# Folded weight product in quarters over all attention steps, four load buffers, and an earlier last-stage load

## The chip, the cores and the metric

The kernel runs on one core of a Trainium2 chip. The metric is the device time of one execution in microseconds (us), here the median of three runs. Engines are named as the profile names them: PE (matrix products), DVE and ACT (element-wise work), POOL (GpSimd), SP (the queue that issues the DMAs).

## The reference

A decaying causal attention over 8 batches of 8 heads, 576 positions and head size 64, then two three-layer networks on the 4608 resulting tokens:

```
scores = scale * q @ k.T
ret    = scores * Dmat            # Dmat = gamma_head ** (i - j) for i >= j, else 0
x      = (ret @ v), heads side by side            # 4608 x 512
h      = max(max(x @ w1, x @ w2), x @ w3)         # 512 -> 768
x2     = h @ w_out                                # 768 -> 512
a, b   = x2 @ u1, x2 @ u2                         # 512 -> 1024
out    = ((a * b) @ u3) @ uo                      # 1024 -> 1024 -> 512
```

All inputs and outputs are 32-bit floats.

## The kernel before, in words

**Numbers.** Each large product is made from operands split into a high part (a cast, on ACT: `chi`, `whi`, `u3hi`, `uohi`) and a low part (the rest, on DVE: `clo`, `wlo`, `u3lo`, `uolo`). Three matmuls hi*hi, hi*lo and lo*hi go into one sum. The two layers after the product a*b are one: the kernel multiplies u3 by uo itself while attention runs (the folded weight product, `wcst` and `wcd`), and the last stage uses the result.

**Attention** takes 32 steps, each for one batch and two heads. A step n has `scores(n)` (16 + 4 small matmuls), `sum_state(n)`, and for step n-1 `query_state` and `values`. DVE weighs the scores (`probs`, L709 and L713) and makes the running state (L725, L728). POOL scales values and queries (`vdec`, `qdec`, L499). ACT copies the result out (`xst`, L582), and SP stores it to `xd`. The inputs of a step come in two loads of 576 KB, `qks` (two buffers) and `vks` (three). The folded product is eight blocks of 24 matmuls (L912 to L914), one in every second step from step 3 to step 17, between `scores` and `query_state`. Beside that, weights 0 to 4 of the first network stage are loaded, summed (POOL) and split within attention, and so are all seven blocks of the first token tile.

**The network stages** B, C, I, O (512 to 768, 768 to 512, 512 to 1024, 1024 to 512) take six token tiles each. A tile is cut into 2x2 blocks and multiplied by seven products P1 to P7 in place of eight; for it POOL makes four sums of token blocks (`raw`) and four of weight blocks (`wraw`). The loop variable `it` counts units, that is one weight for one tile: B has 54 (it 0 to 53), C 12, I 48 (it 66 to 113), O 12 (it 114 to 125). In iteration `it` PE runs in this order: P1(it), P5(it-1), P4(it-1), P6(it), P3(it-1), P2(it), P7(it). Every product first waits for what its operands need: the low part of its token block (`c_lo`) in the first unit of a tile, the low parts of its weight (`w_lo`) in the first tile of a stage. ACT copies P1's bank (`s`), P6's (`u`) and P7's (`w`) out of the accumulator; DVE adds P2, P3 and P5 to them.

**Order.** All engines run fixed lists. The tables HI_STD, HI_CI, HI_IO (ACT) and LO_STD, LO_CI, LO_IO (DVE) say after which point of an iteration each of a tile's seven blocks is split, around the end of one tile ("end") and the first unit of the next ("next"). W_LOAD_AT, W_SUM_AT, W_SPLIT_AT, RAW_AT and T_AT give the iteration at which SP, POOL and the splitters take up a weight or a tile. W_FREE and SLOT_FREE say which product must be done before a memory range is used again. The weights of stage O are numbers 19 and 20 (units it 114 and 115 for the first tile), its first tile is number 18; those of stage B are 0 to 8.

## Time and profile before

| | before |
|---|---|
| median of three runs | 1333.28 us (1332.85 to 1336.16) |
| profiled execution, its own time | 1333.16 us |
| its span | 1331.4 us |
| PE busy | 1259.7 us (95%) |
| DVE, ACT, POOL busy | 803.4, 459.7, 452.3 us |
| granted PE clock, mean | 0.982 |
| attention, to PE's first product of stage B | 235.5 us |

PE is busy nearly all the time, so the time can only fall where PE waits or where its clock is lowered. A row of the timeline has a start, a duration, the engine, the line, the operation, written tile and read tiles, and in brackets how long the engine had been idle before and what ended that.

### The profile page before, as it was taken

To read this page: it belongs to the slowest core of one execution; us is meant where nothing else is said; L and a number is where in the kernel's file an instruction comes from. 1 tells how busy PE (TensorE), PEld (TensorE's weight loads), DVE (VectorE), ACT (ScalarE), POOL (GpSimd) and SP (SyncE) were. 2 spreads that over 40 slices of the span, in tenths; PEclk is the share of its full clock that TensorE was granted. 3 is DMA by queue.
4 is the path that set the end of the run, shared out by engine and by line. 5 is a ranking of instruction groups with operands and counts; after the bars stand their busy time and mean duration, and the time that the engine had idled before them with its cause. 6 is when DMAs were issued, how large, how long until landed. Compare 5 with 4: busy or idle time off the path is not lost.

```text
span 1331.4 us, 20535 instructions
## 1 busy us (share of the span) xinstructions
PE 1259.7 (95%) x8032; PEld 1235.0 (93%) x8032; DVE 803.4 (60%) x1194; ACT 459.7 (35%) x707; POOL 452.3 (34%) x248
## 2 busy tenths in 40 slices
PE   6999878999999999999999999999999998499999
PEld 5888867999999999999899999999999997499999
DVE  5555668656455555548889677454535537756762
ACT  2112112433333232325455444232323323344442
POOL 2333566602020202006598562202012007635550
PEclk8999988999999999999999999999999999799999
DMA  8778786302020202031655541313313133334441
GB/s 312 235 239 288 252 286 223 133 29 95 25 95 31 89 31 90 31 137 54 224 180 176 174 157 53 109 48 101 104 58 102 52 130 120 130 137 148 155 142 66
DMA packets 82929, 174.37 MB, mean 131 GB/s; under 512 B 8976, under 2 KB 57488, under 8 KB 82832
## 3 DMA queue, kind: packets, MB, share of 16 engines
q1 hardware_dynamic: 82832, 173.05, 37.9%
q8 instruction: 64, 1.05, 0.3%
q14 instruction: 33, 0.27, 0.1%
HBM read 109.58 MB, written 63.44 MB: 130 GB/s over the span
## 4 chain that ended last, share of the span: by engine, by line
PE 74%; DMA 10%; DVE 9%; issue 4%; POOL 1%; SPq 1%; ACT 1%; DVEq 0%; POOLq 0%
PE ps L944 23%; PE ps L945 23%; PE ps L946 23%; DVE clo L699 3%; DMA vks<-vk 3%; DMA u3raw<-u3T 2%; DVE wlo L699 2%; DMA x2d<-h 2%; DMA gd<-h 1%; PE ps L890 1%; PE ps L875 1%; PE ps L900 1%; DVE state L728 1%; DVE probs L709 1%; POOL qdec L499 1%
## 5 line engine op out<-in xcount | busy, mean ns | idle before, releaser
L944 PE MATMUL ps<-chi,whi 128*128 128x384 f32 x2016 | 678.7, 337 | 32.4 <-DVE wlo L699 15.3
L945 PE MATMUL ps<-clo,whi 128*128 128x384 f32 x2016 | 676.4, 336 | 0.0
L946 PE MATMUL ps<-chi,wlo 128*128 128x384 f32 x2016 | 676.3, 335 | 0.0
L499 POOL TENSOR_TENSOR raw<-raw,raw 128x768 f32<-128x768 f32 (+2 forms) x96 | 273.3, 2866 | 536.7 <-DMA raw<-xd 222.0
L944 PEld LDWEIGHTS ps<-chi,whi 128*128 128x128 f32 x2016 | 380.7, 189 | 37.9 <-issue 18.6
L945 PEld LDWEIGHTS ps<-clo,whi 128*128 128x128 f32 x2016 | 380.9, 189 | 0.0
L946 PEld LDWEIGHTS ps<-chi,wlo 128*128 128x128 f32 x2016 | 380.7, 189 | 0.0
L699 DVE TENSOR_TENSOR clo<-raw,chi 128x768 fp32r<-128x768 f32 (+2 forms) x168 | 259.5, 1567 | 16.5 <-ACT chi L622 16.1
L622 ACT CAST chi<-raw 128x768 fp32r<-128x768 f32 (+2 forms) x168 | 180.7, 1081 | 93.8 <-PE ps L946 86.6
L689 ACT COPY w<-ps 128x384 f32<-128x384 f32 x126 | 60.8, 482 | 253.7 <-PE ps L946 252.2
L675 ACT COPY u<-ps 128x384 f32<-128x384 f32 x126 | 60.8, 482 | 168.1 <-PE ps L946 166.6
L816 DVE TENSOR_TENSOR h<-ps,u 128x384 f32<-128x384 f32 x66 | 36.7, 556 | 122.3 <-PE ps L946 122.3
L789 DVE TENSOR_TENSOR h<-ps,w 128x384 f32<-128x384 f32 x66 | 36.7, 556 | 119.9 <-PE ps L946 97.3
L656 ACT COPY s<-ps 128x384 f32<-128x384 f32 x126 | 60.7, 482 | 69.5 <-PE ps L946 69.0
L499 POOL TENSOR_TENSOR wraw<-w,wraw 128x256 f32<-128x256 f32 (+2 forms) x21 | 23.1, 1102 | 177.0 <-DMA w<-wC 80.4
L789 DVE TENSOR_TENSOR w<-ps,w 128x384 f32<-128x384 f32 x60 | 33.4, 556 | 82.4 <-PE ps L946 82.4
L699 DVE TENSOR_TENSOR wlo<-wraw,whi 128x768 fp32r<-128x768 f32 (+4 forms) x42 | 80.9, 1926 | 2.9 <-ACT whi L607 2.7
L499 POOL TENSOR_TENSOR qdec<-qks,qtab 128x512 f32<-128x512 f32 x32 | 42.0, 1314 | 77.3 <-PE ps L890 77.3
L582 ACT COPY xst<-ps 128x576 f32<-128x576 f32 x32 | 20.4, 639 | 132.0 <-PE ps L900 132.0
L816 DVE TENSOR_TENSOR u<-ps,u 128x384 f32<-128x384 f32 x60 | 33.3, 555 | 53.3 <-PE ps L946 53.3
L667 ACT COPY h<-ps 128x384 f32<-128x384 f32 x66 | 31.7, 480 | 96.3 <-PE ps L946 82.2
L499 POOL TENSOR_TENSOR vdec<-vks,vtab 128x512 f32<-128x512 f32 x32 | 42.6, 1330 | 46.0 <-DMA vks<-vk 45.2
(41 smaller groups left out, 917.1 us busy)
## 6 DMA issues: line engine op xcount, KB each, us to landing
qks<-qk SPq DMA_DIRECT2D x32, 576.0 KB, 4.4
vks<-vk SPq DMA_DIRECT2D x32, 576.0 KB, 6.0
gd<-h SPq DMA_DIRECT2D x96, 192.0 KB, 1.9
raw<-gd SPq DMA_DIRECT2D x24, 768.0 KB, 7.2
hd<-h SPq DMA_DIRECT2D x72, 192.0 KB, 1.9
raw<-hd SPq DMA_DIRECT2D x24, 576.0 KB, 5.7
raw<-xd SPq DMA_DIRECT2D x24, 384.0 KB, 5.4
x2d<-h SPq DMA_DIRECT2D x48, 192.0 KB, 2.5
```

Of the source, the lines that this page charges most:

```text
L499: return nc.gpsimd.tensor_tensor(out_, a, b, op)
L622: nc.scalar.copy(chi[st][pos][:, :, :], raw_block(tau, pos)[:, :, :]).then_inc(c_hi, 1)
L656: nc.scalar.copy(sbuf_s[it % 2][:, :], ps[:, X[it % 2], 0:N]).then_inc(s_made, 1)
L667: nc.scalar.copy(H[1][0][:, :], ps[:, X[g % 2], 0:N]).then_inc(copied21, 1)
L675: nc.scalar.copy(sbuf_u[it % 2][:, :], ps[:, X[it % 2], 0:N]).then_inc(u_made, 1)
L689: nc.scalar.copy(sbuf_w[it % 2][:, :], ps[:, X[it % 2], 0:N]).then_inc(w_made, 1)
L699: return nc.vector.tensor_tensor(out_, whole, hi.bitcast(f32), ALU.subtract)
L789: nc.vector.tensor_tensor(to[:, :], ps[:, Z[g % 2], 0:N], sbuf_w[g % 2][:, :], ALU.add).then_inc(sum22, 1)
L816: nc.vector.tensor_tensor(to[:, :], ps[:, Z[g % 2], 0:N], sbuf_u[g % 2][:, :], ALU.add).then_inc(sum12, 1)
L944: nc.tensor.matmul(to, w1, x1, start=(start and k == 0), stop=False, skip_group_check=True)
L945: nc.tensor.matmul(to, w1, x2, start=False, stop=False, skip_group_check=True)
L946: last = nc.tensor.matmul(to, w2, x1, start=False, stop=(k == KH[st] - 1), skip_group_check=True)
```

## The change

The folded product no longer comes in eight blocks but in 32 quarters of 6 matmuls: one in each step from 2 to 31, and the last two in step 32. The splits of u3 and uo and the copies out are spread to match. `qks` and `vks` get four buffers each and are loaded three steps ahead, `qdec` gets two buffers. The memory for this comes from moving things: the `vks` buffers lie where token blocks 4 to 6 of the first tile go, so these are split in iteration 0 of stage B; and only weights 0 and 1 are prepared within attention, while 2 to 8 are loaded, summed and split in iterations 0 to 6. DVE makes the state after the extra splits of a step, not before. In the last stage, tile 18 is loaded at iteration 107 in place of 110 and its first two sums stand at 109 in place of 112, weights 19 and 20 stand otherwise too, at other addresses. In stages C and O, block 6 of a tile has one buffer in place of two and is loaded last, apart from the other three, and these three are issued after two of the stores of the iteration, not before. The tables for the splits are spread by one or two points.

```
-HI_IO = {("end", "s"): [0], ("end", "u"): [1], ("end", "p2"): [2], ("next", "p5"): [3],
-         ("next", "p3"): [4, 5, 6]}
-LO_STD = {("end", "21"): [0], ("end", "11"): [1, 2], ("next", "start"): [3], ("next", "22"): [4],
-          ("next", "21"): [5], ("next", "12"): [6]}
...
-LO_IO = {("end", "21"): [0], ("end", "11"): [1, 2], ("next", "22"): [3], ("next", "12"): [4, 5],
-         ("next", "11"): [6]}
+HI_IO = {("end", "s"): [0], ("end", "u"): [1], ("end", "p3"): [2], ("end", "p2"): [3],
+         ("next", "p5"): [4], ("next", "p3"): [5, 6]}
+LO_STD = {("end", "21"): [0], ("end", "12"): [1], ("end", "11"): [2], ("next", "22"): [3],
+          ("next", "21"): [4], ("next", "12"): [5], ("next", "11"): [6]}
...
+LO_IO = {("end", "21"): [0], ("end", "12"): [1], ("end", "11"): [2, 3], ("next", "22"): [4],
+         ("next", "11"): [5, 6]}
...
-    O: [(112, P4), (112, P3), (113, P2), (113, P5), (113, P3), (113, P3), (113, P3)],
+    O: [(111, P3), (112, P3), (112, P3), (113, P2), (113, P5), (113, P3), (113, P3)],
...
-          19: ((109, P3), 18), 20: ((111, P3), 0)}
+          19: ((107, P3), 0), 20: ((110, P3), 18)}
-W_LOAD_AT = {6: 0, 7: 1, 8: 2, 9: 49, ... 18: 69, 20: 112}
-W_SUM_AT = {5: 0, 6: 1, 7: 2, 8: 3, 9: 50, ... 19: 111, 20: 113}
-W_SPLIT_AT = {wi: it + 1 for wi, it in W_SUM_AT.items()}
+W_LOAD_AT = {2: 0, 3: 0, 4: 0, 5: 1, 6: 2, 7: 3, 8: 4, 9: 49, ... 18: 69, 19: 109, 20: 112}
+W_SUM_AT = {2: 0, 3: 1, 4: 2, 5: 3, 6: 4, 7: 5, 8: 6, 9: 50, ... 19: 110, 20: 113}
+W_SPLIT_AT = {wi: it + (wi >= FIRST_W[C]) for wi, it in W_SUM_AT.items()}
...
-        _a = {C: 48, I: None, O: 110}[_st]
-        T_AT[_tau] = {C: (50, 51), I: (65, 65), O: (112, 113)}[_st]
+        _a = {C: 48, I: None, O: 107}[_st]
+        T_AT[_tau] = {C: (50, 51), I: (65, 65), O: (109, 110)}[_st]
...
-WC_AT = {3 + 2 * kb: kb for kb in range(FT2)}
+WC_FROM = 2
+def quarters(n):
+    if n == NP:
+        return range(NP - WC_FROM, QUARTERS)
+    return range(n - WC_FROM, n - WC_FROM + 1) if n >= WC_FROM else ()
+U3_LOAD = {max(4 * kb - 2, 0): kb for kb in range(1, FT2)}
+U3_HI = {max(4 * kb, 1): kb for kb in range(FT2)}
+U3_LO = {max(4 * kb + 1, 1): kb for kb in range(FT2)}
+UO_AT = {1: 0, 2: 1, 3: 2, 4: 3}
+P1_W_LOAD = {8: 0, 10: 1}
+P1_W_SUM = {10: 0, 12: 1}
+P1_RAW = 12
+P1_T = {15: 0, 16: 1, 17: 2, 18: 3}
+P1_HI = {18: 0, 19: 1, 20: 2, 22: 3}
...
             def load_qk(n):
-                if n >= 2:
-                    sp.wait_ge(scored, n - 1)
-                    sp.wait_ge(q_decayed, n - 1)
+                if n >= 4:
+                    sp.wait_ge(scored, n - 3)
+                    sp.wait_ge(q_decayed, n - 3)
             def load_vk(n):
-                if n >= 3:
-                    sp.wait_ge(valued, n - 2)
+                if n >= 4:
+                    sp.wait_ge(valued, n - 3)
...
-                if 2 <= wi <= 5:
+                if 2 <= wi <= 8:
+                    sp.wait_ge(valued, NP)
                     sp.wait_ge(wc_done, FT2)
...
+            def load_raw_rest(tau):
+                sp.wait_ge(c_lo, 7 * tau)
+                load_raw_block(tau, 6)
...
             for it in range(G + 1):
-                if it in RAW_AT:
-                    load_raw(RAW_AT[it])
+                tau = RAW_AT.get(it)
+                two_parts = tau is not None and tau // TILES in (C, O) and tau % TILES
+                if tau is not None and not two_parts:
+                    load_raw(tau)
                 g = it - 1
                 if g >= 0 and ends(g):
...
                         store(g, 1, 0)
+                        if two_parts:
+                            load_raw(tau)
                         sp.wait_ge(sum12, g + 1)
                         store(g, 0, 1)
...
+                if two_parts:
+                    load_raw_rest(tau)
...
+                    elif tau == O * TILES:
+                        pool.wait_ge(prod, DONE[(108, P3)])
...
                 if tau == 0:
-                    if pos == 6:
-                        act.wait_ge(valued, 30)
+                    if pos > 3:
+                        act.wait_ge(valued, NP)
...
+            def wc_quarter(i):
+                kb, part = divmod(i, 4)
+                if part == 0:
+                    pe.wait_ge(u3_lo, kb + 1)
+                    if kb:
+                        pe.wait_ge(wc_out, kb)
...
             for n in range(STEPS):
                 if n < NP:
                     scores(n)
-                if n in WC_AT:
-                    wc_block(WC_AT[n])
+                for i in quarters(n):
+                    wc_quarter(i)
```

**PE in attention.** First before: the end of a block (the last of its 24 matmuls), the rest of that step, and the step behind it, which has none.

```order
L914 MATMUL ps<-uohi_230,u3lo_236 128x512
L890 MATMUL ps<-qdec_249,state_250 128x128 x3
L890 MATMUL ps<-qdec_249,state_250 128x64
L875 MATMUL ps<-vdec_248,vks2_243 128x128 x4
L900 MATMUL ps<-probs_244,vks1_242 64x128 x8
L900 MATMUL ps<-probs_244,vks1_242 64x64 x2
L860 MATMUL ps<-qks_240 128x128 x8
L865 MATMUL ps<-qks_240 128x64 x2
L890 MATMUL ps<-qdec_249,state_250 128x128 x3
L890 MATMUL ps<-qdec_249,state_250 128x64
L875 MATMUL ps<-vdec_248,vks0_241 128x128 x4
```

And now: one step of the changed kernel, the first with a quarter.

```order
L875 MATMUL ps<-qks2_240 128x128 x8
L880 MATMUL ps<-qks2_240 128x64 x2
L930 MATMUL ps<-uohi_228,u3hi1_232 128x512
L932 MATMUL ps<-uolo_229,u3hi1_232 128x512
L934 MATMUL ps<-uohi_228,u3lo1_234 128x512
L930 MATMUL ps<-uohi_228,u3hi1_232 128x512
L932 MATMUL ps<-uolo_229,u3hi1_232 128x512
L934 MATMUL ps<-uohi_228,u3lo1_234 128x512
L905 MATMUL ps<-qdec1_252,state_253 128x128 x3
L905 MATMUL ps<-qdec1_252,state_253 128x64
L890 MATMUL ps<-vdec_250,vks2_244 128x128 x4
L915 MATMUL ps<-probs_246,vks1_243 64x128 x8
```

Every step from 2 on now has six matmuls of the folded product in it, where every second step had 24 or none.

**ACT where stage B begins.** Before, from the last token block of tile 0 to the end of iteration 1; `s0`, `u0`, `w0` belong to iteration 0, `s1` to iteration 1.

```order
L622 CAST chi0_6_62<-raw0_6_55 128x768
L656 COPY s0_223<-ps 128x384
L675 COPY u0_225<-ps 128x384
L689 COPY w0_227<-ps 128x384
L656 COPY s1_224<-ps 128x384
L667 COPY h10_221<-ps 128x384
L675 COPY u1_226<-ps 128x384
L607 CAST whi5_155<-wraw5_157 128x768
```

And now, from the last copy of the folded product on:

```order
L619 COPY wcst_237<-ps 128x512
L673 COPY s0_221<-ps 128x384
L642 CAST chi0_4_60<-raw0_4_53 128x768
L642 CAST chi0_5_61<-raw0_5_54 128x768
L692 COPY u0_223<-ps 128x384
L642 CAST chi0_6_62<-raw0_6_55 128x768
L627 CAST whi2_141<-wraw2_143 128x768
L706 COPY w0_225<-ps 128x384
L627 CAST whi2_141<-wraw2_143 128x1024
L673 COPY s1_222<-ps 128x384
```

Three token casts and both casts of weight 2 have come between the copies that PE waits for in iterations 0 and 1.

**POOL ahead of stage O.** The sums of weights 19 and 20 and of tile 18's token blocks, before:

```order
L499 TENSOR_TENSOR wraw19_213<-w21_19_214,wraw19_213 128x512
L499 TENSOR_TENSOR wraw19_213<-wraw19_213,w21_19_214 128x512
L499 TENSOR_TENSOR wraw19_213<-wraw19_213 128x512 x2
L499 TENSOR_TENSOR raw3_4_117<-raw3_3_116,raw3_0_113 128x1536
L499 TENSOR_TENSOR raw3_1_114<-raw3_6_119,raw3_4_117 128x1536
L499 TENSOR_TENSOR wraw20_217<-w21_20_218,wraw20_217 128x512
```

And now:

```order
L517 TENSOR_TENSOR raw3_4_116<-raw3_3_115,raw3_0_112 128x1536
L517 TENSOR_TENSOR raw3_1_113<-raw3_6_118,raw3_4_116 128x1536
L517 TENSOR_TENSOR wraw19_211<-w21_19_212,wraw19_211 128x512
L517 TENSOR_TENSOR wraw19_211<-wraw19_211,w21_19_212 128x512
L517 TENSOR_TENSOR wraw19_211<-wraw19_211 128x512 x2
L517 TENSOR_TENSOR raw3_3_115<-raw3_6_118,raw3_3_115 128x1536
L517 TENSOR_TENSOR raw3_5_117<-raw3_2_114,raw3_1_113 128x1536
L517 TENSOR_TENSOR wraw20_215<-w21_20_216,wraw20_215 128x512
```

Weight 20's sums now stand last, behind all four token sums; before, two token sums stood behind them.

## Rows read from the trace of the kernel before

**Rows 1.** What PE waited for, first 300 us (total, times, longest).
```profile
PE ps L875 <- POOL vdec L499: 14.9, 8, 5.8
```

**Rows 2.** PE timeline in attention.
```profile
15.97 1.21 PE L900 MATMUL ps<-probs,vks 128*64 128x128 f32 x20
21.27 2.08 PE L860 MATMUL ps<-qks 64*128 64x128 f32 x16 [4.09 <-DMA qks<-qk]
...
68.12 1.16 PE L860 MATMUL ps<-qks 64*128 64x128 f32 x16
72.50 1.16 PE L860 MATMUL ps<-qks 64*128 64x128 f32 x16
...
87.86 1.16 PE L860 MATMUL ps<-qks 64*128 64x128 f32 x16
94.77 1.00 PE L890 MATMUL ps<-qdec,state 128*128 128x128 f32 x8
97.78 1.16 PE L860 MATMUL ps<-qks 64*128 64x128 f32 x16
```

**Rows 3.** DMA in 0 to 240 us.
```profile
DMA packets 27518, 62.18 MB, mean 259 GB/s; under 512 B 2823, under 2 KB 15968, under 8 KB 27495
```

**Rows 4.** The page: DMA issues, size, median us from issue to landing.
```profile
vks<-vk SPq DMA_DIRECT2D x32, 576.0 KB, 6.0
raw<-gd SPq DMA_DIRECT2D x24, 768.0 KB, 7.2
```

**Rows 5.** Windows in attention; the last two numbers: DMA share, GB/s.
```profile
56.00:60.00 4.00, 3.94 (x52) 3.61 (x52) 2.35 (x10) 1.13 (x2) 2.55 (x2) 1.00 0.90 292
184.00:188.00 4.00, 1.54 (x7) 1.54 (x8) 0.00 (x0) 0.00 (x0) 2.86 (x4) 0.50 1.04 412
```

**Rows 6.** Timelines of SP, POOL, ACT at stage B's start.
```profile
237.23 0.37 SPq L384 DMA_DIRECT2D wraw<-wB  x1
...
241.37 0.74 POOL L499 TENSOR_TENSOR wraw<-w,wraw 128x256 f32<-128x256 f32 x1 [6.49 <-DMA w<-wB]
244.27 0.73 POOL L499 TENSOR_TENSOR wraw<-w,wraw 128x256 f32<-128x256 f32 x1
...
236.92 0.48 ACT L656 COPY s<-ps 128x384 f32<-128x384 f32 x1
241.93 0.48 ACT L656 COPY s<-ps 128x384 f32<-128x384 f32 x1 [0.56 <-PE ps L946]
248.54 1.05 ACT L607 CAST whi<-wraw 128x1024 fp32r<-128x1024 f32 x1
```

**Rows 7.** PE timeline in stage C, at two tile starts.
```profile
702.59 0.45 PE L944 MATMUL ps<-chi,whi 128*128 128x384 f32 x1 [1.29 <-DVE h L789]
...
726.06 0.45 PE L944 MATMUL ps<-chi,whi 128*128 128x384 f32 x1 [1.33 <-DVE h L789]
```

**Rows 8.** ACT timeline, `s` of iterations 109, 110, 116, 117 and `w` of 115.
```profile
1082.22 0.48 ACT L656 COPY s<-ps 128x384 f32<-128x384 f32 x1 [0.56 <-PE ps L946]
1089.50 0.48 ACT L656 COPY s<-ps 128x384 f32<-128x384 f32 x1 [0.56 <-PE ps L946]
...
1176.64 0.48 ACT L689 COPY w<-ps 128x384 f32<-128x384 f32 x1 [0.54 <-PE ps L946]
1178.72 0.48 ACT L656 COPY s<-ps 128x384 f32<-128x384 f32 x1 [0.22 <-PE ps L946]
...
1193.28 0.48 ACT L656 COPY s<-ps 128x384 f32<-128x384 f32 x1 [1.60 <-PE ps L946]
```

**Rows 9.** PE timeline, waits between stages I and O.
```profile
1101.90 0.59 PE L944 MATMUL ps<-chi,whi 128*128 128x384 f32 x1 [2.04 <-DVE h L789]
...
1152.12 0.66 PE L944 MATMUL ps<-chi,whi 128*128 128x384 f32 x1 [9.86 <-DVE wlo L699]
...
1166.12 0.66 PE L944 MATMUL ps<-chi,whi 128*128 128x384 f32 x1 [5.43 <-DVE wlo L699]
```

**Rows 10.** The chain of waits after the row at 1101.90 (start, us).
```profile
1105.05 0.32 PE ps L944
```

**Rows 11.** DVE and POOL timelines around stage O's start and later.
```profile
1135.06 4.56 DVE L699 TENSOR_TENSOR clo<-raw,chi 128x1536 fp32r<-128x1536 f32 x1
...
1158.64 0.56 DVE L789 TENSOR_TENSOR h<-ps,w 128x384 f32<-128x384 f32 x1 [6.67 <-PE ps L946]
1175.03 5.26 DVE L699 TENSOR_TENSOR clo<-raw,chi 128x1536 fp32r<-128x1536 f32 x3
...
1186.71 16.96 POOL L499 TENSOR_TENSOR raw<-raw,raw 128x1536 f32<-128x1536 f32 x4 [24.55 <-DMA raw<-gd]
```

240 lines of the change are left out of this document (112 added, 128 removed).

## The prediction

> **What bounds the kernel now.** I read first what PE waited for, then PE's timeline where it waited. PE is the bound: the table of times has it busy for 95% of the span, so I looked only for its gaps and its slow stretches. Three places have them: attention (to 237 us), stage C (small), and the passage from stage I to stage O. Elsewhere PE hardly pauses, and an iteration takes 1089.50 - 1082.22 = 7.28 us in stage I and 1193.28 - 1178.72 = 14.56 us in stage O [rows 8].
>
> In attention PE waited mostly for POOL's scaled values, 14.9 us [rows 1], which waited for `vks`, and once 4.09 us for `qks` [rows 2]. A step without a block takes 72.50 - 68.12 = 4.38 us. A step with one takes 97.78 - 87.86 = 9.92, so a block costs 5.54, a quarter of it 1.39 [rows 2]. If PE never waited, 32 steps and 8 blocks would take 140.2 + 44.3 = 184.5 us; they take 237.
>
> Between I and O, from the `s` copy of iteration 109 to the `w` copy of 115, 94.42 us pass [rows 8]. Undisturbed, from the two paces (a product is a seventh of an iteration, 1.04 and 2.08): four iterations of I, 29.12; six products of I and one of O, 8.32; four products of O and three of I, 11.44; six products of O, 12.48. Sum 61.36, so 33.1 us are lost. Two waits for weight 20's low parts are 15.3 of it [rows 9]. DVE is late there because its work runs slow beside POOL: a `clo` of 128x1536 took 4.56 us, while three of the same took 5.26 together (1.75 each) when POOL was idle [rows 11]. The `clo`s come ahead of the `wlo` in its list.
>
> **Attention.** Removed are the waits for loads. `vks` takes 6.0 us to land [rows 4]; it is now issued two full steps and a part ahead, over 12 us, so only bandwidth can make it late. The first steps: values(0) started at 15.97 and, with the 1.1 us that it lasts, step 2 can start at 17.1, where it waited 4.09 us for `qks` and started at 21.27 [rows 2]. The uo loads that were ahead of this load in the queue are now spread behind it. From 17.1 on, 30 steps have one quarter each: 4.38 + 1.39 = 5.77, and I add 0.1 for each change between the small attention tiles and the full ones, since there are 31 such places now instead of 8: 5.87 x 30 = 176.1. That gives 193.2. Step 32 has two quarters (2.9) and query and values (97.78 - 94.77 = 3.01 with sum_state, about 2 without): 198.1 [rows 2]. Then ACT copies x and the last block, which PE waits for, 1.4 by the durations of such copies: PE starts stage B at 199.5 and the first `s` is at 200.9, where it was at 236.92 [rows 6]. I add 2 us for loads that come late in bursts: 203. Gain 34.
>
> The extra work beside PE has room in a step of 5.87. POOL has two operations of about 1.3 each, DVE under 4 us and at most one split more in a step; since the state is made after the splits, a split moves it, but PE wants it only after the next scores and a quarter. The quarters of one block wait for `u3lo` only at the first of four.
>
> On the 0.1: the Trainium skill, TensorEngine Tiling (Array Packing), section Key Properties, says that a change of tiling mode, not just of tile, drains the engine. It gives no price. If the drain were 0.5 us at each of the 23 new places, the sum would be some 9 us higher (at no drain 3 us lower); the block's 5.54 above already holds one entry and one exit, and a quarter's entry is all that is added, so the trace speaks for little.
>
> **Start of stage B.** Added: weights 2 to 4 are loaded only once attention is done, and ACT's casts of weight 2 stand ahead of the `s` copy of iteration 1. Reckoned from PE's start p: two stores, then SP issues the load at p + 0.9. Before, issue to POOL's first sum took 241.37 - 237.23 = 4.1, and the four sums 244.27 - 241.37 = 2.9 [rows 6]. So the sums are done at p + 7.9, the cast (1.05 [rows 6]) at p + 9.0, and the copy starts there. Undisturbed it stood 241.93 - 236.92 = 5.0 after the first `s`, that is p + 6.4. Late by 2.6; after such a gap the clock is low (after the 2.04 us wait at 1101.90 [rows 9] matmuls still came 0.32 us apart at 1105.05 [rows 10], where 7.28 us for 42 of them make 0.173; some 3.5 us at 1.2 GHz, a cost of 1.8). What is queued behind the waiting cast on ACT is just this copy, and PE's P6(1) waits for it. Cost 4, bounds 0 (the load is quicker) and 12 (DVE, slowed by POOL, makes iterations 1 to 4 late too). Later weights come one an iteration, 2.9 us of POOL in 7.28: hidden.
>
> **Stage C.** The stores of h now go ahead of the next tile's loads; the waits of 1.29 and 1.33 at tile starts [rows 7] ended on a store, so they go. Gain 2.5, bounds 0 and 3.
>
> **Stage I to O.** Tile 18 is loaded three iterations (22 us) earlier. Its first two sums on POOL can be done about 1090 in old time (the second waits for P3 of 108), weight 19's by 1096, the last two by 1104, weight 20's by 1113. P1 of 113 starts about 1110. So POOL is idle while DVE splits, and a `clo` costs 1.75 rather than 4.56. What then is late is DVE itself. From T, P1(113)'s start, it gets its first sum at T + 2.1 and has 11 sums of 0.56, seven `clo` and the first `wlo` of weight 20 at 1.75 [rows 11]: 6.2 + 14.0 = 20.2, with 1 us of waits T + 23.3. PE wants it for P1(115) at T + 7.3 + 11.5 = T + 18.8. So 4.5 us are still lost, 2.2 for the low clock after it, 1 at the second `wlo`, and I give 1.4 for contention that I overlook: 9 of 33.1 remain. Gain 24. Bounds: 10, if DVE's operations are as slow as before in half of them, and 30.
>
> **Block 6 with one buffer** (stages C and O): cost 0, covered by POOL's slack and a whole iteration. In O the last `clo` of a tile ends some 15 us into its first iteration; load 7.2 (it was four of them together) [rows 4], sum 16.96 / 4 = 4.24, cast 1.5, `clo` 1.75 [rows 11]: 29.7, and P6 of the next tile is at 29.1 + 6.2 = 35.3. The waits of the new ACT and DVE order lie inside this slack.
>
> **Sum.** -34 + 4 - 2.5 - 24 = -56.5. From the profiled execution's 1333.16: 1276.7; it lies 0.12 under the median, so I forecast 1277.
>
> **Rivals.**
> 1. *The DMA engines become attention's bound.* 62.18 MB move in the first 240 us [rows 3], less some 2.6 for weights that are now later: 59.5 MB, in 199 us 299 GB/s. For: with stores in the mix a window reached 292 at a share of 0.90 [rows 5]. Against: loads alone reached 412 at full share. At 290, 205 us plus the start of 2: 8 us later, with cold clocks after the waits 10: 1287.
> 2. *The passage to O stays long*, since DVE still meets POOL (weight 20's sums, or tile 19's loads). Then only the waits before iteration 115 go, some 11 us in place of 24: 1290. For: both `wlo` waits are the largest and come at the end of DVE's list, which has the same work. Against: POOL is free there by my times. Trainium skill, Trainium Architecture — The Big Picture, section What this means for kernel authors: the port pair that DVE and GpSimd share is an exclusive lock, not a split of bandwidth. The 4.56 against 1.75 agrees with a long wait for such a lock, and by that rule any overlap that stays costs in full.
> 3. *Stage B starves on weights 2 to 8*: each of five or six iterations loses 1.5 to 2 us to splits slowed by POOL: 1287.
> 4. *Slower than before.* Block 6 comes late at each of ten tile starts in C and O: its chain above is 5.6 us short of the deadline. With the slow `clo` (4.56, +2.8), the wait of the last `clo` (+2.8) and ACT held behind the cast, it is due; it decides from 5.6 us a tile on (56 / 10), and at 8 with cold clocks it costs 80: 1357. Against: it needs all slow ends at once, and POOL starts after the load.
>
> **Chances.** Forecast 0.60, rival 1 0.16, rival 2 0.12, rival 3 0.07, rival 4 0.03; 0.02 for a loss elsewhere that leaves the time about where it was. Range 1264 to 1298: below by the lower bounds (attention without the 2, passage 30, start 0: 1265), above by rivals 1 or 2 with half of another. Less than 0.3% (4 us) can't be told from no change: faster 0.95, same 0.02, slower 0.03.
>
> **What would show it.** Right: first `s` copy of stage B at 200 to 205 us, steps of 5.8 to 6.0, no wait for `vdec` or `qks`; one wait of 2 to 3 us at P6 of iteration 1; `clo` of 128x1536 near 1.8 us at iterations 113 and 114 and one wait of 4 to 5 us for `wlo` before iteration 115. Wrong: DMA share near 1.0 through attention with PE waiting for loads; steps over 6.1 us without a wait (the drain); waits for `clo` at tile starts in C and O.

## The result, and the profile after

| | before | after |
|---|---|---|
| median | 1334.72 us (4 runs, 1332.85 to 1337.61) | 1279.09 us (4 runs, 1278.05 to 1280.15) |
| ratio | | 0.9581, 95% interval 0.9559 to 0.9603 |
| profiled execution, its span | 1331.4 us | 1276.7 us |
| PE busy | 1259.7 us (95%) | 1245.4 us (98%) |
| granted PE clock, mean | 0.982 | 0.996 |

The change took 56 us off, 4.2%; 1277 was forecast. Where the 54.7 us of the span went is seen from marks that both kernels have: ACT's `s` copy of an iteration, and its `w` copy of iteration 115.

| stretch | before | after | difference | forecast |
|---|---|---|---|---|
| start to `s` of iteration 0 (attention) | 236.92 | 199.57 | -37.35 | -34 |
| to `s` of 5 (start of stage B) | 34.95 | 36.49 | +1.54 | +4 |
| to `s` of 54 (rest of B) | 358.75 | 358.92 | +0.17 | 0 |
| to `s` of 66 (stage C) | 135.57 | 136.07 | +0.50 | -2.5 |
| to `s` of 109 (stage I) | 316.03 | 315.67 | -0.36 | 0 |
| to `w` of 115 (I to O) | 94.42 | 75.23 | -19.19 | -24 |
| to the end | 154.76 | 154.75 | -0.01 | 0 |

What PE waited for in the whole of the changed kernel, the largest four (view of waits: in total, times, longest):

```profile
PE ps L965 <- DVE wlo L716: 9.5, 2, 5.7
PE ps L965 <- DVE h L804: 6.4, 6, 2.0
PE ps L875 <- DMA qks<-qk: 4.4, 1, 4.4
PE ps L890 <- POOL vdec L517: 3.5, 1, 3.5
```

The 14.9 us of waits for `vdec` in attention [rows 1] have become one of 3.5. That one and the 4.4 for `qks` are the very first loads, before 10.3 us.

**Attention.** PE's timeline, from `scores(1)` on, and three later steps:

```profile
12.29 2.08 PE L875 MATMUL ps<-qks 64*128 64x128 f32 x16
...
18.66 1.16 PE L875 MATMUL ps<-qks 64*128 64x128 f32 x16
...
19.93 0.50 PE L930 MATMUL ps<-uohi,u3hi 128*128 128x512 f32 x1
20.26 0.40 PE L932 MATMUL ps<-uolo,u3hi 128*128 128x512 f32 x1
...
87.94 1.16 PE L875 MATMUL ps<-qks 64*128 64x128 f32 x16
...
93.71 1.16 PE L875 MATMUL ps<-qks 64*128 64x128 f32 x16
...
198.23 0.41 PE L965 MATMUL ps<-chi,whi 128*128 128x384 f32 x1 [1.39 <-issue]
```

A row with brackets would be a wait; between 12.29 and 198.23 there is none. (The last row's 1.39 "issue" is the end of attention: PE waits for ACT to copy the last block out, 1.4 in the forecast.) Where step 2 once waited 4.09 us for `qks` [rows 2] it now starts at 18.66, and each step from then on takes 5.77 us (93.71 - 87.94, and 5.77 or 5.78 in each of the others from step 2 to 30): 4.38 of a step without a block and 1.39 of a quarter.

The DMA engines carried that with little to spare. A window of attention before (the columns are PE, PEld, DVE, ACT, POOL busy, then granted clock, DMA share, GB/s):

```profile
10.00:50.00 40.00, 35.67 (x306) 32.21 (x307) 22.20 (x58) 9.79 (x12) 12.37 (x10) 0.91 0.78 282
```

and after:

```profile
10.00:50.00 40.00, 39.72 (x399) 36.37 (x400) 30.15 (x82) 10.30 (x13) 19.76 (x16) 1.00 0.97 364
50.00:100.00 50.00, 50.00 (x542) 45.59 (x543) 34.21 (x102) 11.93 (x17) 28.01 (x26) 1.00 0.99 348
100.00:150.00 50.00, 50.00 (x533) 45.53 (x531) 36.83 (x100) 12.29 (x18) 28.27 (x21) 1.00 0.90 290
```

A share of 0.97 to 0.99 stands beside a PE that is busy for the whole window: with the loads three steps ahead of their use, a late one has room. From 100 us on the rate falls, and PE is busy all the same.

**Start of stage B.** ACT's timeline, with the cast of weight 2 ahead of the `s` copy of iteration 1, and PE's row that waits for this copy:

```profile
199.57 0.48 ACT L673 COPY s<-ps 128x384 f32<-128x384 f32 x1 [1.55 <-PE ps L967]
...
206.92 1.04 ACT L627 CAST whi<-wraw 128x1024 fp32r<-128x1024 f32 x1 [2.09 <-POOL wraw L517]
207.87 0.47 ACT L673 COPY s<-ps 128x384 f32<-128x384 f32 x1
...
208.39 0.44 PE L965 MATMUL ps<-chi,whi 128*128 128x384 f32 x1 [1.78 <-ACT s L673]
208.67 0.34 PE L966 MATMUL ps<-clo,whi 128*128 128x384 f32 x1
```

The copy is 8.30 us after that of iteration 0, where it was 5.01 [rows 6]. PE lost 1.78 us, and the next matmul takes 0.34: the clock stayed at its upper level (2.4 GHz). It does not do so in every profile. Eight of the kernels profiled here have this wait at 1.76 to 1.83 us. In three (this one, e1_blocks and e2_late) the clock stayed up, and the stretch from the first `s` to `s` of 5 takes 36.49 to 36.51. In five (e3, e4, e7, e11, e12) ten matmuls soon behind it came 0.32 us apart, and the stretch takes 38.04 to 38.13. PE in e4_uo_first, the wait and the first slow matmul:

```profile
211.52 0.45 PE L963 MATMUL ps<-chi,whi 128*128 128x384 f32 x1 [1.77 <-ACT s L671]
...
212.74 0.52 PE L963 MATMUL ps<-chi,whi 128*128 128x384 f32 x1
```

**Stage C.** The waits of 1.29 and 1.33 [rows 7] are still there, a little shorter; one of three tile starts in PE's timeline (the next two, at 690.11 and 713.28, waited 1.03 and 1.05):

```profile
666.94 0.45 PE L965 MATMUL ps<-chi,whi 128*128 128x384 f32 x1 [1.05 <-DVE h L804]
```

DVE's own waits in this stage have changed. In the kernel before (635 to 795 us):

```profile
DVE h L789 <- DMA x2d<-h: 6.9, 4, 3.5
DVE h L789 <- DMA gd<-h: 3.8, 1, 3.8
...
DVE clo L699 <- ACT chi L622: 2.9, 4, 1.9
```

and in the changed one (600 to 760 us), where no wait for a store is left:

```profile
DVE clo L716 <- ACT chi L642: 17.6, 6, 4.9
```

PE's waits follow neither of them closely. In the kernel before, DVE was not waiting for a store ahead of the two rows [rows 7]: it came to the sum `h` straight from a `clo`, without a pause. Its waits for stores stand elsewhere (1.31 at 712.08, for one). DVE before, and DVE now ahead of the wait at 666.94:

```profile
701.99 0.55 DVE L789 TENSOR_TENSOR h<-ps,w 128x384 f32<-128x384 f32 x1
```

```profile
663.04 3.37 DVE L716 TENSOR_TENSOR clo<-raw,chi 128x1152 fp32r<-128x1152 f32 x1
```

POOL was summing token blocks at that time; a `clo` of this size alone takes 1.35. So the `clo` that is queued ahead of `h` is slow, and the late cast before it (DVE stood 2.91 us for it, to 660.02) may add to that. The e7_c_two_buffers run below takes the late cast away. PE's waits over the whole stage sum to 6.4 us before and 6.6 now. A wait of 2.01 at 621.67, at the stage's first tile, is the longest there.

**From stage I to O.** The waits of 2.04, 9.86 and 5.43 us [rows 9], and three more of 1.55, 2.40 and 3.04 between the first two, have become two:

```profile
1097.48 0.41 PE L965 MATMUL ps<-chi,whi 128*128 128x384 f32 x1 [3.75 <-DVE wlo L716]
...
1111.33 0.66 PE L965 MATMUL ps<-chi,whi 128*128 128x384 f32 x1 [5.75 <-DVE wlo L716]
```

The second one comes off DVE, which meets POOL there. DVE's and POOL's timelines:

```profile
1103.53 0.56 DVE L804 TENSOR_TENSOR h<-ps,w 128x384 f32<-128x384 f32 x1 [6.20 <-PE ps L967]
1104.01 1.75 DVE L716 TENSOR_TENSOR clo<-raw,chi 128x1536 fp32r<-128x1536 f32 x1
1105.67 5.51 DVE L716 TENSOR_TENSOR wlo<-wraw,whi 128x2048 fp32r<-128x2048 f32 x1
...
1104.08 13.87 POOL L517 TENSOR_TENSOR raw<-raw,raw 128x1536 f32<-128x1536 f32 x3 [1.99 <-DMA raw<-gd]
```

DVE had been idle for 6.20 us. Then it does a `clo` of the *next* tile first, and after it the `wlo` that PE waits for, which takes 5.51 us beside POOL's sums; the same operation alone took 2.28 (weight 19's, at 1071.14). The seven `clo` of tile 18 take 1.71 to 1.76 each, 12.1 us in all. Before they took 19.9: the 4.56 of [rows 11] was the slowest, the others had 2.37, twice 3.88, and three times 1.7.

### The profile page after: what moved, and what is told of

The parts are those of the page before. It is cut to its first block, busy times and chain, and to the rows that moved or that the text cites. A ratio compares the mean times of both kernels' runs of the same rounds, so it can differ in the third digit from the quotient of the medians.

```text
span 1276.7 us, 20538 instructions
## 1 busy us (share of the span) xinstructions
PE 1245.4 (98%) x8032; PEld 1223.4 (96%) x8032; DVE 784.2 (61%) x1194; ACT 458.6 (36%) x707; POOL 443.0 (35%) x248
## 3 DMA queue, kind: packets, MB, share of 16 engines
q8 instruction: 64, 1.05, 0.3%
## 4 chain that ended last, share of the span: by engine, by line
PE 46%; DVE 2%; issue 2%; DMA 1%; ACT 1%; SPq 0%; DVEq 0%; ACTq 0%
PE ps L965 15%; PE ps L967 15%; PE ps L966 15%; DMA gd<-h 1%; DVE clo L716 1%; DVE wlo L716 1%; ACT chi L642 0%; DVE h L804 0%; DVE h L851 0%; ACT w L706 0%; DVE h L857 0%; SPq L400 0%; DVE s L851 0%; DVE h L831 0%; DVE h L811 0%
## 5 line engine op out<-in xcount | busy, mean ns | idle before, releaser
L517 POOL TENSOR_TENSOR raw<-raw,raw 128x768 f32<-128x768 f32 (+2 forms) x96 | 261.4, 2743 | 594.9 <-DMA raw<-xd 207.8
L716 DVE TENSOR_TENSOR wlo<-wraw,whi 128x768 fp32r<-128x768 f32 (+4 forms) x42 | 63.5, 1512 | 3.0 <-POOL wraw L517 2.9
L726 DVE TENSOR_TENSOR probs<-ps,dec 128x512 f32<-128x512 f32 x64 | 41.3, 687 | 18.0 <-PE ps L880 18.0
```

The source lines that it names most:

```text
L517: return nc.gpsimd.tensor_tensor(out_, a, b, op)
L716: return nc.vector.tensor_tensor(out_, whole, hi.bitcast(f32), ALU.subtract)
L726: nc.vector.tensor_tensor(probs[:, n % 2, h, 0:NC * CH].rearrange("p (n c) -> p n c", c=CH), ps[:, h, :].rearrange("p (n c) -> p n c", c=C ...
```

## The experiments

Each kernel is the changed one with the edit shown. "First `s`" is ACT's `s` copy of iteration 0, at 199.57 in the changed kernel, and "the passage" runs from `s` of 109 to `w` of 115, 75.23 there. In the other profiles with the same code in the passage it takes 74.97 to 79.34; one way to that difference is shown at e6_w20. So attention's edits are judged by first `s`, each from one profile. How well it repeats: the seven kernels that have the changed attention (after, e5 to e8, e10, e11) have it at 198.78 to 199.57.

### What in the change sped up attention

**e1_blocks**: whole blocks again, at steps 5, 9, ... 29 and 32.

```
-    return range(n - WC_FROM, n - WC_FROM + 1) if n >= WC_FROM else ()
+    return range(n - 5, n - 1) if n % 4 == 1 and n >= 5 else ()
```

> The changed kernel with one thing undone: the folded product comes again in whole blocks of 24 matmuls, one in every fourth step (5, 9, ... 29, 32); four buffers and all else stay. Theory (the buffers did it, PE has no reason to wait once loads are three steps ahead): PE has the same work, 4.38 us a step and 5.54 a block, so the first s copy of stage B stays at 200 to 203 us and the time at 1279 to 1283. Rival (the even spreading did it): between blocks the loads have to come at 1.44 MB in 4.38 us, 329 GB/s, and DVE and POOL have only 4.38 us a step; PE waits again, s copy at 212 or later, time 1290 or more.

**e2_late**: the loads two steps ahead, with the waits of the old buffers.

```
-                if n >= 4:
-                    sp.wait_ge(scored, n - 3)
-                    sp.wait_ge(q_decayed, n - 3)
+                if n >= 3:
+                    sp.wait_ge(scored, n - 1)
+                    sp.wait_ge(q_decayed, n - 1)
...
-                if n >= 4:
-                    sp.wait_ge(valued, n - 3)
+                if n >= 3:
+                    sp.wait_ge(valued, n - 2)
...
-                if n + 3 < NP:
-                    load_qk(n + 3)
+                if 3 <= n + 2 < NP:
+                    load_qk(n + 2)
...
-                if n + 3 < NP:
-                    load_vk(n + 3)
+                if 3 <= n + 2 < NP:
+                    load_vk(n + 2)
```

> The changed kernel with one thing undone: quarters and four buffers stay, but each load is issued only two steps ahead and behind the waits of the kernel before (qks behind scores and scaled queries of n - 1, vks behind values of n - 2), as if there were two and three buffers. Theory (the early issue did it): vks is issued about 6.6 us before POOL needs it and takes 6.0 us to land in the median, so PE waits for vdec in many steps; s copy at 207 to 217 us, time 1286 to 1296. Rival (spreading did it): a step of 5.77 us leaves enough time for a load; s copy at 200 to 202, time 1279 to 1281.

**e3_blocks_late**: both edits at once.

> Both undone: blocks of 24 and late issue. This is close to attention as it was (s copy at 236.9 us), but without three weights prepared in it. Theory that the two parts add up: the loss is the sum of the losses of the two single undoings. Rival, that each alone hides what the other would cost: the loss is much larger than the sum, s copy at 225 to 235 us, time 1305 to 1315.

**e4_uo_first**: the four loads of uo ahead of `qks` and `vks` of step 2, as before.

```
             load_u3(0)
-            load_uo(0)
+            for i in range(4):
+                load_uo(i)
             load_qk(2)
             load_vk(2)
-            load_uo(1)
...
-                if n in (1, 2):
-                    load_uo(n + 1)
```

> The changed kernel with the four uo loads ahead of the third qks load again, as before. Theory: step 2 waits for qks until about 21 us, as before (4.09 us there), and nothing after it can win that back since PE is busy without a gap from there: time +3 to +4.5, 1282 to 1283.5. Rival: later steps had slack and absorb it: no change.

| | median us | ratio to before | first `s` | later by |
|---|---|---|---|---|
| e1_blocks | 1287.01 | 0.9645 (0.9614 to 0.9676) | 203.20 | 3.6 |
| e2_late | 1286.08 | 0.9642 (0.9613 to 0.9672) | 203.94 | 4.4 |
| e3_blocks_late | 1297.32 | 0.9720 (0.9682 to 0.9757) | 214.76 | 15.2 |
| e4_uo_first | 1284.55 | 0.9628 (0.9596 to 0.9661) | 202.69 | 3.1 |

By first `s`, going back to blocks alone, or to late loads alone, costs about 4 us. Both together cost 15.2, nearly twice the 8.0 that the two would sum to. The medians are a weaker witness: 7.9, 7.0 and 18.2 us over the changed kernel's, which is 3.3 more than a plain sum, about as much as the intervals allow. Some 4 us of each of the three lie in the passage, 78.88 to 79.34 in their profiles, which attention's edits don't touch. None of these three expectations was met in full: e1 was 4 us over its time; e2's `s` lies between its theory (207 or later) and its rival (202 at most); for e3 the sum of the parts was too little and the rival's 225 too much.

The waits of e1_blocks, and then of e3_blocks_late, up to 245 us (the waits in the very first loads are left out for e1, and 3.6 us of them are in e3's 12.5):

```profile
PE ps L905 <- DVE state L745: 4.1, 8, 1.3
```

```profile
PE ps L890 <- POOL vdec L517: 12.5, 9, 3.6
```

With blocks and early loads only DVE's state is late, a little at a time. With blocks and late loads it is POOL's `vdec` again, as in the kernel before [rows 1], and the state as well (3.9). The start of the steps around e3's third block shows where: step 12 began at 78.26, step 13 (with the block) at 85.38, that is 7.12 us in place of 4.38, step 14 at 95.27. Steps without a block are over sooner (4.38) than a load lands (6.0 [rows 4]), so the lead is used up ahead of the next block. e4's steps are as expected, its time is 1 us over: step 2 starts at 20.25 in place of 18.66, and step 3 at 27.55 in place of 24.43.

15.2 and 3.1 are less than half of the 37.35. My reason for the rest was that weights 2 to 4 no longer load within attention. **e9_old_queue** puts back more of the old order: e3 and e4 together, SP's stores of the folded product ahead of the `vks` load, and POOL's wait for the one `qdec` buffer. The blocks stand in steps 5, 9, ... 29 and 32, as in e3, not in steps 3 to 17 as before, and DVE's state stays behind the splits.

```
+                if n - 1 in WC_READ:
+                    store_wc(WC_READ[n - 1])
                 if n in P1_W_LOAD:
...
                     store_x(n - 1)
-                if n - 1 in WC_READ:
-                    store_wc(WC_READ[n - 1])
...
-                if n >= 2:
-                    pool.wait_ge(queried, n - 1)
+                if n >= 1:
+                    pool.wait_ge(queried, n)
```

> Attention nearly as before: blocks and late issue as in the run with both undone (s copy at 214.8 us), and also the uo loads first, the stores of the folded product ahead of the vks load in SP's list, and the scaled queries waiting for the query product of the step before. What stays changed is that only two weights in place of five are prepared within attention, and the state after the splits. Theory (the rest of the 37 us is mostly the work and loads of the three weights moved out, not the queue's order): s copy at 218 to 222 us, by the 3.1 us of the uo loads and a few for the rest; time 1299 to 1303. Rival (queue order and the single buffer of scaled queries are what cost): s copy at 228 to 236, time 1310 to 1318.

Measured: 1322.64 (1314.06 to 1325.41), ratio 0.9898 (0.9862 to 0.9935), first `s` at 235.22, before 236.92; the profiled execution was its shortest. Its waits up to 245 us:

```profile
PE ps L888 <- POOL vdec L515: 17.9, 8, 4.1
PE ps L873 <- DMA qks<-qk: 12.2, 8, 4.3
```

The whole gain of attention is gone although the three weights are still out of it. So blocks, late loads, the queue's order and the one buffer can cost all 37 us by themselves (the rival's 228 to 236 for `s`; the time lies even above its 1318), and my theory, that mostly the weights did, fell. That moving the weights saved nothing is not shown, though. In the kernel before, the twelve steps from 19 to 31 (149.52 to 226.69) had no block, and the three weights in them; undisturbed they take 52.6 us, and they took 77.2. PE waited 10.7 us for `vdec` there, and POOL 22.9 us for `vks`; the longest two:

```profile
186.46 2.08 PE L875 MATMUL ps<-vdec,vks 128*128 128x128 f32 x8 [5.79 <-POOL vdec L499]
...
185.14 1.26 POOL L499 TENSOR_TENSOR vdec<-vks,vtab 128x512 f32<-128x512 f32 x1 [7.90 <-DMA vks<-vk]
```

So 24.6 us were lost in these steps before. In e9 the same steps (137.93 to 219.82), with three blocks and no weights, lost 12.7; e9 lost more in the steps up to 19 instead, 28.3 for 17.7. Since the blocks stand elsewhere, no run here separates the weights' share. The `qdec` buffer can be tried by itself. **e12_one_qdec** is e3_blocks_late with the last of the edits above alone.

> Blocks and late issue as in the run with both undone (s copy at 214.8 us), and of the three further things of the run before last (s copy at 235.2) only one: the scaled queries of step n wait for the query product of n - 1, as with one buffer. SP's order and the uo loads stay as changed. Theory (this wait makes POOL hold the qks load and the next scaled values behind the query product, so it is the main part): s copy at 225 to 233 us, time 1304 to 1312. Rival (SP's order and the uo loads were the 20 us): s copy at 215 to 219, time 1294 to 1300.

Measured: 1314.21 (1311.40 to 1322.14), ratio 0.9845 (0.9815 to 0.9874), against 0.9720 of e3: 1.25% of 1333 or 17 us for the one buffer. That is the theory's side, with the time 2 us over its range. (The profiled execution was its longest, first `s` at 238.25, 23.5 later than e3's; 17 is the better number.) POOL's timeline in it:

```profile
105.01 1.27 POOL L517 TENSOR_TENSOR qdec<-qks,qtab 128x512 f32<-128x512 f32 x1 [5.08 <-PE ps L905]
```

POOL stands 5.08 us at `qdec` until PE has done `query_state`, which stands behind a whole block. The next `vdec` is queued behind it, and so is the release of `qks`, on which the next load waits. So the buffer wait of one small operation makes a load late, and POOL then waits for `vks` (1.97 us at 112.63). By first `s`, one thing missing costs 4 us and two cost 15; by the ratios, the third adds 17, and SP's order and uo another 7 (0.9898 against 0.9845; the two intervals overlap a little). Each covers for the others. What `qdec` would cost alone, with quarters and early loads in place, wasn't tried.

### The passage from stage I to O

**e5_o_late**: tile 18 loaded at iteration 110 and summed at 112 and 113, as before.

```
-        _a = {C: 48, I: None, O: 107}[_st]
-        T_AT[_tau] = {C: (50, 51), I: (65, 65), O: (109, 110)}[_st]
+        _a = {C: 48, I: None, O: 110}[_st]
+        T_AT[_tau] = {C: (50, 51), I: (65, 65), O: (112, 113)}[_st]
```

> The changed kernel with tile 18's loads at iteration 110 and its sums at 112 and 113 again (POOL's order as before: weight 19, two token sums, weight 20, two token sums); addresses, tables and weight loads as changed. Theory (the gain between I and O is POOL being done before DVE splits): the low parts of tile 18 take 3 to 4.6 us again and most of the 19.2 us gained from s(109) to w(115) is lost: time 1290 to 1298. Rival (the new tables or the earlier freed memory gave it): within 3 us of 1279.

Measured: 1290.30, ratio 0.9665 (0.9627 to 0.9704), passage 88.38. So the early load is 9 to 13 of the 19.2 us, and by subtraction the other 6 (94.42 - 88.38) belong to all else that was changed there (tables, addresses, the earlier weight 19), which was not tried apart. The time is as the theory had it, the way to it only in part: of tile 18's seven `clo` just one was slow (4.16), and one sum of DVE (3.27 at 1089.45, where such a sum takes 0.55 alone), both beside POOL's sums. PE's longest waits from 1060 to 1150 us:

```profile
PE ps L965 <- DVE wlo L716: 12.0, 2, 8.4
PE ps L965 <- DVE w L804: 3.9, 1, 3.9
```

**e6_w20**: weight 20's low parts earlier in DVE's list (and its casts in ACT's): the first after point "22" of iteration 114, the second right behind block 5 of tile 18, ahead of the last `clo` and of tile 19. Block 4's `clo` goes one place back for it. The lines that put these splits later are taken out.

```
-LO_IO = {("end", "21"): [0], ("end", "12"): [1], ("end", "11"): [2, 3], ("next", "22"): [4],
+LO_IO = {("end", "21"): [0], ("end", "12"): [1], ("end", "11"): [2, 3], ("next", "21"): [4],
...
+                if it == 114 and point == "22":
+                    split_weight(20, 0)
                 for tau, pos in due(LO_STD, LO_CI, LO_IO, it, point):
                     split_tokens(tau, pos)
+                    if it == 114 and pos == 5:
+                        split_weight(20, 1)
```

> The changed kernel with weight 20's splits moved up at iteration 114: its first part ahead of token blocks 4 to 6, its second between blocks 5 and 6, on ACT and DVE. No work is added or removed. Theory (the two waits that are left there, 3.75 and 5.75 us, are only the order of DVE's list, the second made worse by POOL's sums of tile 19): both go, and the low clock after them, gain 9 to 12 us, time 1267 to 1270. Rival (DVE has too much work there in any order): the waits move to clo of blocks 4 to 6 at P5, P4 or P3 of 114, gain under 4.

Measured: 1269.66, ratio 0.9514 (0.9483 to 0.9545), passage 67.32. The whole of PE's waits from 1060 to 1150 us:

```profile
PE ps L973 <- ACT w L710: 2.1, 1, 2.1
PE ps L973 <- DVE h L812: 1.2, 1, 1.2
```

Both waits for `wlo` are gone, the time is within the expectation, and the granted clock is 1.00 from 1090 to 1114 us (0.79 in the 8 us behind the 2.1 us wait). DVE's timeline shows why: both low parts are done early and alone (2.29), and it is now a `clo`, for which PE has time, that meets POOL:

```profile
1094.30 2.29 DVE L720 TENSOR_TENSOR wlo<-wraw,whi 128x2048 fp32r<-128x2048 f32 x1
...
1098.63 4.61 DVE L720 TENSOR_TENSOR clo<-raw,chi 128x1536 fp32r<-128x1536 f32 x1
```

How the same code can take 75 us in one profile and 79 in another is seen at the same place in e1_blocks, PE and then DVE:

```profile
1102.05 0.66 PE L965 MATMUL ps<-chi,whi 128*128 128x384 f32 x1 [3.74 <-DVE wlo L716]
...
1119.49 0.66 PE L965 MATMUL ps<-chi,whi 128*128 128x384 f32 x1 [8.25 <-DVE wlo L716]
...
1109.68 4.25 DVE L716 TENSOR_TENSOR clo<-raw,chi 128x1536 fp32r<-128x1536 f32 x1
```

The first wait is the same (3.74 and 3.75). Behind it e1's matmuls come 0.32 us apart from 1102.50 to 1107.94, 5.4 us at the lower clock level (1.2 GHz); in the changed kernel the first six still come 0.18 apart, and only those from 1098.62 to 1102.09, 3.5 us, are slow. DVE's next sum, which waits for PE's product, came 7.15 us after the wait in e1 (1109.20) and 6.05 here (1103.53). By then POOL was at work in e1, the `clo` took 4.25 in place of 1.75 (the `wlo` 5.50, as there), and the second wait was 8.25 in place of 5.75.

**e11_pool_wait** tests the contention by itself: POOL begins tile 19's sums only when weight 20's second low part is done. DVE's order stays.

```
                 if i == 0:
+                    if tau == 19:
+                        pool.wait_ge(w_lo, 42)
```

> The changed kernel, where POOL additionally waits with the sums of tile 19 until both low parts of weight 20 are done; no work is moved on any other engine, the order of DVE's list is as changed. Theory (the second wait is POOL and DVE in each other's way): the last low part takes 2.3 us in place of 5.5 and the clo before it 1.8, the wait before P6 of 115 falls from 5.75 to 8 us to about 2.5, w(115) - s(109) to 70 to 73 us, time 1273 to 1277 (if tile 19 isn't late for it). Rival (DVE's order alone): wait as before, 1279 or more, since POOL starts later.

Measured: 1275.62, ratio 0.9555 (0.9525 to 0.9586), passage 71.51. PE, DVE and POOL there:

```profile
1109.19 0.41 PE L967 MATMUL ps<-chi,whi 128*128 128x384 f32 x1 [2.52 <-DVE wlo L718]
...
1106.76 2.29 DVE L718 TENSOR_TENSOR wlo<-wraw,whi 128x2048 fp32r<-128x2048 f32 x1
...
1109.12 15.54 POOL L517 TENSOR_TENSOR raw<-raw,raw 128x1536 f32<-128x1536 f32 x4 [27.33 <-DVE wlo L718]
```

With POOL away `wlo` takes 2.29, and the wait falls from 5.75 to 2.52: 3.2 of it was contention. The other 2.5 I put down to DVE's order, a `clo` (1.75) ahead of the `wlo`; e6, which changes the order, has no such wait. Wait, passage and time are all as the theory said.

### Block 6 in stage C, and the fastest version

**e7_c_two_buffers**: in stage C block 6 has two buffers again and is loaded with the rest.

```
-            return raw[tau // TILES][pos]
+            st = tau // TILES
+            return raw[st][7 if pos == 6 and st == C and tau % 2 else pos]
...
-                    if pos != 6 or t == 0 or st in (B, I):
+                    if pos != 6 or t == 0 or st != O:
                         load_raw_block(tau, pos)
...
-                if two_parts:
+                if two_parts and tau // TILES == O:
                     load_raw_rest(tau)
```

> The changed kernel with two buffers for token block 6 in stage C again, loaded together with the other three (still behind the two stores). Theory (the stores ahead of the loads did remove the wait for a store, but the late block 6 made a new one of 1.05 us at three tile starts, by POOL's sum, ACT's cast and DVE's list): those three waits go, gain about 3 us, time 1276. Rival: the waits stay, since POOL and DVE slow each other in any case: no change.

Measured: 1279.80, ratio 0.9582 (0.9545 to 0.9618), no different in time. Stage C (from `s` of 54 to `s` of 66) takes 134.22. PE's wait that answers to the one of 1.05 at 666.94 is 0.87, the next two are 0.86. DVE's wait for the casts in 600 to 760 us, and the `clo` ahead of `h` at that tile start:

```profile
DVE clo L718 <- ACT chi L644: 6.4, 3, 2.8
```

```profile
662.43 3.36 DVE L718 TENSOR_TENSOR clo<-raw,chi 128x1152 fp32r<-128x1152 f32 x1
```

DVE waits 6.4 us for casts in place of 17.6, and none of the three waits of PE goes: the theory was wrong there and in the time, and its rival right. What is the same with one buffer and two is the slow `clo`, 3.36 beside POOL, so I put the waits down to it; no run took POOL away there. At most 0.2 of each goes with the late casts. By time alone the case is open. Over all profiles the stage takes 133.87 to 134.22 in the three kernels with two buffers and 135.49 to 137.15 in the ten others that have the changed order, so against e7's 134.22 the single buffer costs between 1.3 and 2.9 us. **e8_w20_c** is e6 and e7 together.

> Both of the last two edits together: 1264 to 1267 if both gains are real and add up; a version faster than both kernels.

Measured: 1268.49, ratio 0.9503 (0.9472 to 0.9534), against 0.9514 of e6: the right sign, within the intervals, and above the 1264 to 1267 that was expected.

**e10_best** adds to e8 that two things of weight 2 come later: ACT's cast of its second part stands behind the `s` copy of iteration 1, and DVE's low part of its first part behind point "22" of that iteration, not in iteration 0. ACT's edit first, then DVE's:

```
+                if it == 1 and point == "s":
+                    split_weight(2, 1)
...
+                if it == 1 and point == "22":
+                    split_weight(2, 0)
```

> The last version (weight 20's splits moved up, two buffers for block 6 in stage C) and the second cast of weight 2 on ACT behind the s copy of iteration 1, its first low part on DVE behind the first sum of that iteration. Theory: the wait of 1.78 us at P6 of iteration 1 was this cast; the first five iterations take 35.0 to 35.3 us instead of 36.5 to 38.1, time 1265 to 1267.5. Rival: the splits of weights 3 and 4 are late then and take it back: no change.

Measured: 1265.64, ratio 0.9490 (0.9466 to 0.9513): the fastest kernel here, some 1% faster than the changed one (0.9581). ACT's `s` copy of iteration 1 (that of iteration 0 starts at 199.25):

```profile
205.82 0.48 ACT L681 COPY s<-ps 128x384 f32<-128x384 f32 x1 [0.56 <-PE ps L981]
```

The copy now waits for PE's product alone (0.56), the cast follows at 207.11, and the copy comes 6.57 us after the first in place of 8.30. `s` of 5 comes 35.99 after the first; 35.0 to 35.3 was expected. With the wait at P6 it takes 36.5 where the clock stays up and 38.1 where it falls, so this last edit is worth 0.5 to 2.1 us by the profiles; its time can't be told from e8's.

## Why the prediction was right, and where not

The forecast of 1277 is closer than its parts are. Against the table above, attention came out 3.4 us better and the start of stage B 2.5 better than forecast, stage C 3.0 worse and the passage 4.8 worse. These misses nearly cancel, and that is luck; the large steps, attention and the passage, were each right within about a fifth.

**Attention, -34 forecast, -37.35 measured.** The steps were right: no wait for loads, step 2 free of the uo loads (e4: 3.1 us), and a step of 4.38 + 1.39. The small terms were off both ways. Step 2 began at 18.66, not at 17.1: `scores(1)` took 2.08 us (1.77 before), and the `query_state` after it 1.97, where it had taken 1.10; the granted clock is given as 1.00 there both times, so the rows don't say why. The forecast took the start of `values(0)` from the trace before, and such a start was not repeated. Against these 1.6 us, two additions of 5 us in all weren't needed. The first of them, 0.1 us a step for the change of tile size, was counted twice. The change exists, and costs about 0.1; but it takes place in a step without a quarter just as well. PE's timeline before, a step without a block, and then the row behind a block's `query_state` (the one at 94.77 [rows 2]):

```profile
69.38 1.10 PE L890 MATMUL ps<-qdec,state 128*128 128x128 f32 x8
70.32 1.11 PE L875 MATMUL ps<-vdec,vks 128*128 128x128 f32 x8
...
95.61 1.11 PE L875 MATMUL ps<-vdec,vks 128*128 128x128 f32 x8
```

`query_state` takes 70.32 - 69.38 = 0.94 us right behind the small tiles of the scores, and 95.61 - 94.77 = 0.84 behind a block. In the changed kernel the quarter's first matmul has the 0.10 (the next starts 20.26 - 19.93 = 0.33 after it, later ones 0.23 apart) and `query_state` is short. So the 0.1 moves, and isn't added. The rule of the Trainium skill (TensorEngine Tiling (Array Packing), Key Properties), that a change of mode drains the engine, may be what these 0.10 us are; it is a fifth of the 0.5 that I had weighed, and no new places were made for it. The 2 us for late bursts weren't lost either. The forecast did not say which part of the change does it, and e9 and e12 show how much it left out: the second `qdec` buffer, which it doesn't speak of, is the largest single part once quarters and early loads are gone. By my theory for e9 I would have named the weights first.

**Start of stage B, +4 forecast, +1.5 measured** (up to +3.2 in the other profiles: 38.13 - 34.95). The mechanism was right, piece by piece: from PE's start at 198.23 the load was issued after 1.25 us (0.9 forecast) and the copy started after 9.64 (9.0). The size was off because PE's wait was 1.78, not 2.6, and the clock did not fall after it in this profile (0.34 for the next matmul), where 1.8 us were put down for that. That term was not wrong in itself: in five of the eight profiles with this wait the clock did fall, and there it cost the 1.6 us between 36.5 and 38.1.

**Stage C, -2.5 forecast, +0.5 measured.** Two steps failed. The first is the reading that the waits of 1.29 and 1.33 [rows 7] ended on a store. DVE's waits for stores, 6.9 + 3.8 us, are gone as forecast, but ahead of these two rows DVE was at a `clo`, not at a store, and the waits stay: 1.05 now, 0.86 in e7. The second is "Block 6 with one buffer: cost 0": 17.6 us at `clo` for the casts took the stores' place, where there were 2.9. It reckoned when PE needs block 6, and not what is queued behind the waiting `clo` in DVE's list. With two buffers in C (e7) the stage is 134.22, 1.35 under the kernel before and not 2.5, and the single buffer thus costs 1.3 to 2.9 us, seen in the profiles only. In stage O, where the same edit was made, nothing is lost (-0.01 us).

**I to O, -24 forecast, -19.2 measured.** Of 33.1 lost us 13.9 stay, not 9. The first wait was forecast at 4.5 and is 3.75. The second `wlo`, forecast at 1, is the mis-sized term: 5.75 us. I had counted DVE's work up to the first low part only. Ahead of the second stands a `clo` of tile 19, and POOL's sums for tile 19 run beside it: 3.2 us contention (e11), the rest order. The forecast's picture of the kernel before was also too even: it took a `clo` at 4.56, and of the seven only one had that, so POOL's absence saved 7.7 us on them. e6, which takes both low parts forward, gets back 7.9 us, and leaves 67.32 against the undisturbed 61.36.

**The rivals.** Rival 1's condition came true, a share of 0.97 to 0.99 over 90 us, and its consequence didn't: the engines delivered 348 to 364 GB/s there, not 290. The window at 0.90 and 292 [rows 5] was no ceiling; the after profile itself has 290 at 0.90 where nothing waits. Nor was the window at 412 one of "loads alone": two stores to `xd`, of 96 and 192 KB, were issued in the 4 us before it and took 8 us to land. Rival 2 was right in part: DVE still meets POOL once, for 3.2 us, not in the whole passage. The rule that it leaned on (Trainium skill, Trainium Architecture — The Big Picture, What this means for kernel authors: a lock and not shared bandwidth) agrees with the rows: a `wlo` of 2.28 alone takes 5.51 beside POOL, more than twice. Rivals 3 and 4 did not come: iterations 0 to 4 took 1.5 us more in all and not in each, stage B from 5 on 0.17, stage C 0.5, and the last stage is 0.01 shorter.

## What to carry to other kernels

Count what is queued behind a waiting instruction, not the waiting instruction alone: the one-buffer `qdec` (17 us by e12), block 6 (1.3 to 2.9 us by e7) and the `clo` of 1.75 us ahead of the `wlo` all cost through what stood behind them. When buffers are short in several places, undoing one tells little, since the others cover for it (4 us each here, 15 for two, 32 for three); test pairs, or start from the version with none. Before you say that a wait ended on a store, look at what the waiting engine's supplier did just ahead of it: in stage C that was a `clo`. And a clock term is worth looking for in several executions: after the same wait it came in five of eight. A low part of a weight that PE needs for a whole new stage goes ahead of token blocks of the next tile, also where DVE has just been idle.

## What the runs showed of the hardware

- The first full-size matmul behind attention's 64-row tiles costs 0.10 us more than the next ones, before and after the change alike.
- DVE beside POOL: `wlo` of 128x2048 2.28 to 2.29 us alone, 5.50 to 5.51 beside POOL's sums; `clo` of 128x1536 1.75 alone, 4.25 to 4.61 beside them; `clo` of 128x1152 1.35 alone, 3.36 to 3.37 beside them.
- Two waits of the same length at the same place, 3.75 and 3.74 us, were followed by 3.5 us of matmuls at PE's lower clock level in one execution, which began only 1.1 us after the wait, and by 5.4 us from its end on in another. What decides it isn't settled by these runs. The same holds at the start of stage B: of eight executions with a wait of 1.76 to 1.83 us three went on at the upper level, and five had ten matmuls 0.32 us apart that began 1.2 to 1.4 us after the wait or, in e12_one_qdec, 0.5 after it. Before, one of 2.04 had been followed by slow matmuls [rows 9, 10].
- PE lost nothing to memory traffic at 0.99 of the DMA engines' time and 348 GB/s in 50 us of mixed loads and stores.
